# Transposing an expert's hidden rows through DMA and VectorE instead of TensorE, in an attention and mixture-of-experts kernel

## The reference, cut to what matters

```python
top2 = np.argpartition(-noisy_logits, 2, axis=1)[:, :2]
...
for e in range(E):
    for k in range(2):
        mask = top2[:, k] == e
        h = np.maximum(x[mask] @ w1[e], 0.0)
        out[mask] += top2_w[mask, k, None] * (h @ w2[e])
```

## Time and profile before

| what | value |
|---|---|
| median of 3 timed executions | 1078.3 us (1078.17 to 1080.13) |
| the profiled execution | 1076.49 us |
| its span, first to last instruction | 1074.7 us |
| TensorE matmul busy | 1062.6 us (99%) |
| VectorE busy | 588.3 us (55%) |
| ScalarE busy | 327.8 us (31%) |
| GpSimd busy | 386.8 us (36%) |
| granted TensorE clock, mean | 1.000 (2.4 GHz) |
| DMA, mean over the span | 124 GB/s |

### The profile page before, as it was taken

One profiled execution on the slowest core, in us unless ns is written; L12 is line 12 of the kernel. 1 busy time (PEld: TensorE's weight loads), 2 busy tenths in 40 slices (PEclk: granted clock), 3 DMA queues, 4 the chain that ended last, 5 costly groups with the idle time before them and its releaser, 6 DMA issues.

```text
span 1074.7 us, 20097 instructions
## 1 busy us (share of the span) xinstructions
PE 1062.6 (99%) x6053; PEld 931.9 (87%) x6054; DVE 588.3 (55%) x1226; ACT 327.8 (31%) x724; POOL 386.8 (36%) x358
## 2 busy tenths in 40 slices
PE   8999999999999999999999999999999999999998
PEld 7878999999999999999988888888888888888886
DVE  6887434363363463453447775565555556555554
ACT  7987122342342432432352111020302021110222
POOL 4667990030030030120185415070706143250486
PEclk9999999999999999999999999999999999999999
DMA  7985525411311311211074536172616344331676
GB/s 218 276 264 190 176 89 187 127 59 30 118 59 30 117 59 30 98 59 30 26 250 153 161 80 174 39 207 46 195 47 161 85 117 127 82 104 39 168 242 235
DMA packets 199634, 133.18 MB, mean 124 GB/s; under 512 B 128752, under 2 KB 161408, under 8 KB 199584
## 3 DMA queue, kind: packets, MB, share of 16 engines
q1 hardware_dynamic: 177728, 75.14, 25.9%
q10 hardware_dynamic: 16032, 38.47, 10.9%
q0 software_dynamic: 5824, 18.95, 5.1%
HBM read 85.87 MB, written 42.73 MB: 120 GB/s over the span
## 4 chain that ended last, share of the span: by engine, by line
PE 93%; POOL 2%; DMA 2%; issue 1%; DVE 1%; SPq 0%; POOLq 0%; ACT 0%; DVEq 0%
PE bank L873 28%; PE bank L1041 20%; PE bank L1062 20%; PE bank L905 14%; PE bank L1075 3%; PE bank L817 2%; PE bank L844 2%; PE bank L827 1%; POOL token_rows_a L750 1%; PE bank L811 1%; DMA token_rows_b<-expert_rows,slots_u 1%; PE bank L958 1%; DMA q_sb<-in_qT 1%; POOL token_rows_a L763 1%; DMA k_sb<-in_kT 0%
## 5 line engine op out<-in xcount | busy, mean ns | idle before, releaser
L873 PE MATMUL bank<-x_parts,mlp_weights 128*128 128x384 f32 x1704 | 309.4, 336 | 0.0
L873 PEld LDWEIGHTS bank<-x_parts,mlp_weights 128*128 128x128 f32 x1704 | 298.3, 188 | 5.3
L1041 PE MATMUL bank<-expert_parts,xT_high 128*128 (+1 forms) x688 | 216.6, 396 | 0.0
L1062 PE MATMUL bank<-expert_parts,hT_high 128*128 (+1 forms) x688 | 212.2, 390 | 0.0
L732 POOL TENSOR_TENSOR expert_parts<-raw_expert_a,expert_parts 128x512 fp32r<-128x512 f32 x64 | 81.4, 1305 | 234.3 <-ACT expert_parts L1372 232.0
L905 PE MATMUL bank<-mlp_weights,hidden_parts 128*128 128x512 f32 x648 | 162.1, 395 | 0.0
L1062 PEld LDWEIGHTS bank<-expert_parts,hT_high 128*128 128x128 f32 x688 | 129.0, 188 | 26.9 <-issue 0.4
L1041 PEld LDWEIGHTS bank<-expert_parts,xT_high 128*128 128x128 f32 x688 | 125.8, 188 | 24.3 <-issue 0.4
L905 PEld LDWEIGHTS bank<-mlp_weights,hidden_parts 128*128 128x128 f32 x648 | 120.2, 188 | 23.4 <-issue 1.0
L1041 PE MATMUL bank<-expert_parts,xT_low 128*128 (+1 forms) x344 | 134.4, 391 | 0.0
L1062 PE MATMUL bank<-expert_parts,hT_low 128*128 (+1 forms) x344 | 134.2, 390 | 0.0
(11 more groups left out here) (220 smaller groups left out, 1230.1 us busy)
## 6 DMA issues: line engine op xcount, KB each, us to landing
raw_expert_a<-in_w ACTq DMA_DIRECT2D x32, 512.0 KB, 4.6
raw_expert_b<-in_w ACTq DMA_DIRECT2D x32, 512.0 KB, 4.2
x_row<-routed_rows SPq DMA_DIRECT2D x172, 64.0 KB, 2.6
expert_rows<-y_row SPq DMA_DIRECT2D x43, 256.0 KB, 2.0
expert_rows<-zeros SPq DMA_DIRECT2D x4, 2304.0 KB, 11.9
v_sb<-in_v SPq DMA_DIRECT2D x32, 256.0 KB, 3.9
q_sb<-in_qT SPq DMA_DIRECT2D x15, 288.0 KB, 3.7
k_sb<-in_kT SPq DMA_DIRECT2D x15, 288.0 KB, 4.1
```

What stands on the lines that cost most here:

```text
L873: last = nc.tensor.matmul(bank[:, 0:CHUNK], w_sb[:, i, wp, at:at + P], xp[:, par, part, k, :], start=n == 0, stop=n == 3 * KB - 1)
L1041: last = nc.tensor.matmul(ps[half][:, 0:512], (xTh, xTl)[xp][:, buf, k, :], ew_sb[:, bass.ds(slot, 1), wp, k * F2 + half * 512:k * F2 + ha ...
L1062: last = nc.tensor.matmul(y_bank(t)[:, 0:D], (hTh, hTl)[hp][:, f, :], ew_sb[:, bass.ds(slot, 1), 2 + wp, f * D:(f + 1) * D].rearrange("p a ...
```

## The change

Tiles 4 to 41 (38 of the 43) no longer have their hidden rows transposed by TensorE:

- `dve_relu` writes `relu` with its columns in another order, so that the blocks for one quarter lie together (still one instruction per half).
- SyncE's queue, `move_hidden(t)`: per half one DMA of 256 KB from `relu` to a new DRAM tensor, and, when that has landed, four DMAs of 64 KB (32 partitions, 4 runs of 512 bytes each) into the new tile `hidden_blocks`. They stand ahead of `load_rows(t + 3)` and `store_rows(t − 1)`. This queue's loop is gone: the 38 tiles are written out.
- `dve_turn`: per half one 32x32-block transpose of 128x512 on VectorE, from `hidden_blocks` into bank 2 or 3, ahead of the hidden split.
- VectorE's order for tile t: split of half 0 of t−1, relu of half 0 of t, split of half 1, relu of half 1, x transposed of t+1, y of t−1.
- TensorE runs, for tile t: up of t, down of t−1. Its loop still has 18 rounds of two tiles, but a round begins between the two halves of a tile's down products, and reads six numbers of the table there and two more between the halves of the next down products.

```diff
+            def move_hidden(t):
+                for half in range(2):
+                    sp.wait_ge(relu_done, 2 * t + half + 1)
+                    sp.dma_start(hs_dram[t % 2, :, half * 512:half * 512 + 512], relu[:, half * 512:half * 512 + 512]
+                                 ).then_inc(hidden_out[half], 16)
+                for half in range(2):
+                    sp.wait_ge(hidden_out[half], 16 * (t + 1 - FIRST_TURNED))
+                    sp.wait_ge(hT_done, 2 * t - 1 + half)
+                    blocks = hs_dram[t % 2, :, half * 512:half * 512 + 512].rearrange("(s r) (q n) -> q r s n", s=BLOCKS, q=BLOCKS)
+                    for q in range(BLOCKS):
+                        sp.dma_start(hB[q * BLOCK:(q + 1) * BLOCK, half * 512:half * 512 + 512].rearrange(
+                            "r (s n) -> r s n", s=BLOCKS), blocks[q]).then_inc(hidden_in[half], 16)
+
+            for t in range(FIRST_TURNED, ETILES - 3):
+                move_hidden(t)
+                load_rows(t + 3, (t + 3) % 2)
+                store_rows(t - 1)
...
-            pe_down2(pe, 3, *fourth)
+            pe_down2(pe, 3, *fourth, (0,))
+
             with pe.Fori(0, (ETILES - 7) // 2) as m:
-                tile(2 * m + 5, 1)
-                tile(2 * m + 6, 0)
...
+                t = 2 * m + 5
+                first, second, third = entries(t - 2), entries(t - 1), entries(t)
+                pe_down2(pe, t - 2, *first, (1,))
+                pe_up2(pe, t, 1, *third)
+                pe_down2(pe, t - 1, *second, (0,))
+                fourth = entries(t + 1)
+                pe_down2(pe, t - 1, *second, (1,))
+                pe_up2(pe, t + 1, 0, *fourth)
+                pe_down2(pe, t, *third, (0,))
...
+        def dve_turn(dve, t, half):
+
+            dve.wait_ge(hidden_in[half], 16 * BLOCKS * (t + 1 - FIRST_TURNED))
+
+            dve.wait_ge(hTl_done, 2 * t - 1 + half)
+            nc.vector.transpose(ps[2 + half][:].rearrange("p (f s c) -> p f s c", s=BLOCKS, c=BLOCK),
+                                hB[:, half * 512:half * 512 + 512].rearrange("p (s f c) -> p f s c", s=BLOCKS, c=BLOCK)
+                                ).then_inc(hT_done, 1)
...
             def tile(t, buf, earlier):
-                dve_hT(dve, t - 1)
-                dve_relu(dve, t)
+                dve_hT(dve, t - 1, (0,))
+                dve_relu(dve, t, (0,))
+                dve_hT(dve, t - 1, (1,))
+                dve_relu(dve, t, (1,))
                 dve_xT(dve, t + 1, buf, earlier)
                 dve_y(dve, t - 1)
```

More of the change, by code:

```diff
@@ L350, in attention_moe_kernel @@
         half_done = sem("half_done")
+        hidden_out = [sem(f"hidden_out_{i}") for i in range(2)]
+        hidden_in = [sem(f"hidden_in_{i}") for i in range(2)]
         y_row_done = sem("y_row_done")
@@ L590, in _ @@
             store_rows(1)
-            with sp.Fori(0, (ETILES - 5) // 2) as m:
-                for a in range(2):
-                    load_rows(2 * m + (5 + a), (5 + a) % 2)
-                    store_rows(2 * m + (2 + a))
-            for t in range(ETILES - 3, ETILES):
-                store_rows(t)
+            load_rows(5, 1)
+            store_rows(2)
+            load_rows(6, 0)
+            def move_hidden(t):
[14 more added lines that the diff above has]
+                store_rows(t - 1)
+            for t in range(ETILES - 3, ETILES - 1):
+                move_hidden(t)
+                store_rows(t - 1)
+            store_rows(ETILES - 2)
+            store_rows(ETILES - 1)
             sp.wait_ge(y_row_out, 16 * ONE + 16 * ETILES)
@@ L1109, in entries @@
                 return entry(pe, t + T_SLOT, 1), entry(pe, t + T_E, E - 1)
-            def tile(t, buf):
-                now = entries(t)
-                before = entries(t - 1)
-                pe_hT(pe, t - 1)
-                pe_up2(pe, t, buf, *now)
-                pe_down2(pe, t - 1, *before)
-                return now
             fourth = entries(3)
```

54 lines of the change are left out of this document (38 added, 16 removed).

## The result

The changed kernel takes **1116.1 us** in the median of 4 executions (1112.3 to 1116.13), the kernel before 1079.2 beside it (4 executions, 1078.17 to 1080.67). The ratio is 1.0332, with a 95% interval of 1.0306 to 1.0358: slower by 3.3%. The forecast was 1079.5 us with a range of 1062 to 1090; the result lies outside it, on the slow side. The profiled execution took 1112.3 us, its span is 1110.5 (before 1074.7) and the mean granted TensorE clock 0.985 (before 1.000).

What follows compares the result with a forecast made beforehand. TensorE, busy 99% of the span, was taken as the bound up to y of tile 37, then GpSimd. 29.9 − 25.2 − 2 − 4 = −1.3 us made the profiled 1076.5 into 1077.8, median 1079.5 us, range 1062 to 1090.

Steps and rivals of the forecast that it cites:

- 29.9 us: TensorE, tiles 4 to 37: removing eight transposes and the refill saves 0.88 us a tile, 34 × 0.88.
- 18 × 1.4 = 25.2 us: TensorE's sequencer: six loads at a round's beginning outlast its 3.7 us lead, stopping the array 1.4 us in 18 rounds.
- hidden by 2.3 us each: VectorE: with two block transposes more a tile, its results still come 2.3 us before TensorE needs them.
- 2 us (1 to 2.5): Tile 5: small sums delay y and the split, so the sequencer is 1.5 us ahead, not 3.7; charged once.
- 6 × (0.2 to 1.7) = 1.5 to 10 us, I take 0.7 each: 4 us: Six weight bursts: half 0's blocks come 0.6 to 2.1 us late, shrinking the sequencer's head start by all above 0.4.
- The array itself does not wait for that: TensorE in bursts: blocks 0.6 to 2.1 us late stay within the array's 2.3 us of cover.
- 7 to 9 us of work in 10.9: SyncE's queue, per tile: all its work with the ten added issues; quiet tiles' trips hidden by 0.5 to 1.4 us.
- The landings in a burst: DMA in weight bursts: y's store lands in 3.9 us; block loads were taken to need 3.5 to 4.2.
- Tiles 38 to 41 ... count for nothing: End of run: their 3.5 us saved on TensorE gain nothing, since GpSimd's chain of 11.16 us per chunk stays.
- The loads stay hidden: Rival, TensorE's sequencer: stops go wholly or partly; 1052 us without any, 1065 with stops half as long; chance 0.23.
- The blocks come late in every tile: Rival, DRAM trip on SyncE's queue: half 0 is 1.1 us too late in 18 rounds, 20 us, 1100 us; chance 0.12.
- Slower: Side of the outcome against the kernel before: chance 0.40, beside faster 0.35 and within 0.2% 0.25.

## Why the prediction was wrong, step by step

- **"29.9 us" for the transposes: right.** Without trip and stops the kernel is 27.3 us faster.
- **"18 × 1.4 = 25.2 us" for six loads: right in mechanism, and in size partly by luck.** The loads cost 23.8 us without the trip and 22.5 with it. Without the trip 15 of the 19 stops were of 0.94 to 0.99 us, 1.2 to 1.3 with the restart of 0.28, against 1.4; three longer ones ahead of y of tile 37 made up for that. With the trip two quiet tiles took 992.08 − 968.37 = 23.71 us, where 23.2 was forecast. In the kernel before the same six loads cost 18.2.
- **Two block transposes on VectorE, "hidden by 2.3 us each": right** as far as the work goes (2.6 us at most).
- **Tile 5, "2 us (1 to 2.5)": right.** y starts at 629.13 us (forecast 629.7). Its stop, at 635.79, is of 2.78 us, 1.3 more than a quiet one: the branch at 633.16 lies 2.6 us ahead of the stop and not 4.1.
- **"6 × (0.2 to 1.7) = 1.5 to 10 us, I take 0.7 each: 4 us" for the bursts: this is the step that failed.** It is all that the prediction charges the trip with. Measured 41 to 42 us for the trip, of which 34 come with the bursts. With 41 in place of 4 the sum is 1079.5 + 37 = 1116.5 us; measured 1116.1, where some of the closeness is luck, since the other terms' errors cancel. The one path that the term has, a shrunk head start of the sequencer, cost 8.6 us, within its own ends. The rest was put at nothing:
  1. **The reads themselves.** The 0.73 us from read to read was taken over from the kernel before. With the trip single reads took up to 1.4 us in place of 0.30, which made the stops 15 us longer. Why is open.
  2. **The clock.** Behind seven stops 12 products ran partly or wholly at half clock: 11.1 us. No row of before had a stop of that length, so this was in no term.
  3. **"The array itself does not wait for that": nearly right.** It waited for the split for 4.5 us, 3.5 of them behind 1087 us.

  Stops 46.7 − 22.8 = 23.9, waits 4.5 and clock 11.1 make 39.5 us, or 38.2 without the 1.3 us of half clock that the run without the trip has as well, against 37.1 between the spans of the two runs (1110.5 − 1073.4).
- **"7 to 9 us of work in 10.9" for SyncE's queue: too small.** The issues were right (3.64 for eight), but the wait for its own store to land and the read of the row's number (0.78) were not counted, and y's store took 0.62 and not 0.4. The round is 10.48 (measured with two loads at a time), and the slack 0.4 and not 2 to 4.
- **The landings in a burst: too short.** There the hidden store landed in 4.0 to 6.7 us (y's store: 3.9, which I took) and the block loads in 4.1 to 5.6 (taken: 3.5 to 4.2).
- **Each tile was reckoned by itself.** The trip is a loop: the queue comes to a tile when it has finished the one before, and relu of t+1 stands behind the turn of t on VectorE. With two loads at a time this hands lateness on to the next burst. In the changed kernel it hardly shows: its stops stretch two tiles to 23.7 us, 11.9 each, and behind each of the five short head starts from 661 to 916 us the next one is full again.
- **"Tiles 38 to 41 ... count for nothing": wrong.** The end no longer hangs on GpSimd's gathers but on TensorE and a late trip: the chain goes through a hidden store of 6.98 us (1077.68) and a block load of 6.05 (1085.97). From y of tile 37 to the end are 65.7 us, 58.7 in the kernel before and 60.2 in the changed kernel without the trip, so most of it is a part of the 41 and not added to it.
- **The rivals.** "The loads stay hidden" fell with the first stop. "The blocks come late in every tile" blamed the trip, rightly, but the head start was short in eight of the 18 stops behind a branch and not in all, and without bursts the trip is hidden until the gathers. Its 1100 us was the nearest of the numbers given, at a chance of 0.12.
- "Slower", at 0.40 the likeliest side, was right for too small a reason.

## What to carry to other kernels

When a change inserts a round trip into a software pipeline, do not ask only whether one trip fits beside one tile. Write down every *loop* it closes (each in-order queue with its waits counted as its time, and each path that returns to its own start one tile later), and compare the longest with the tile's period: what is left is all that a disturbance can be paid back with. If it is little, put the consumer one stage later before anything else is trimmed; here that, with the queue's order and two loads at a time, turned 3.3% slower into 1.6% faster with the same transfers. And a place that reads several numbers into registers has to fit in the sequencer's lead, which any late producer takes away, with room for reads that take longer than they did before the change.

## What the runs showed of the hardware

- In the changed kernel TensorE's granted clock fell behind single stops: after all six of 3.07 to 4.08 us twelve products took 4.4 to 5.5 us in place of 2.72. Of the 13 stops of 1.0 to 2.8 us only one, of 2.40, had this behind it, while two of 2.77 and 2.78 had not. In other runs twelve products took 4.1 us behind a stop of 2.29 (without the trip) and 4.4 behind one of 2.07 (two loads at a time), while behind one of 3.23 us (down products one layer later, at 618.14) the clock stayed at 1.00. So the length of the stop alone does not decide.
- Reading one number of the table into a register took TensorE's sequencer 0.30 us as a rule. In the kernel before and in the run with six loads and no trip it never took more than 0.32 from 620 to 1020 us; in the changed kernel it took up to 1.43.
- The same store of 256 KB landed 2.3 to 2.7 us after its issue in quiet stretches and after 4.0 to 6.7 in bursts (two loads at a time, 670 to 950 us).
- A store of 256 KB took 0.62 us to issue in the queue's rows above where it started within 0.1 us of the last of the four loads of x (y's store in the run with two loads at a time, the hidden store in the one with all x loads between the stores), and 0.34 or 0.43 elsewhere in these rows.
